# Row maxima negated on ScalarE and 1e-9 added on GpSimd, instead of on VectorE, in a top-32 attention with PReLU MLP and switch MoE

## What is computed

```python
scores = scale * np.matmul(q, k.transpose(0, 1, 3, 2))      # (4, 8, 576, 576), scale = 1/8
kth = np.partition(scores, -32, axis=-1)[..., -32:-31]
scores = np.where(scores >= kth, scores, -1000000000.0)
scores = scores - np.max(scores, axis=-1, keepdims=True)
attn = np.exp(scores)
attn = attn / (np.sum(attn, axis=-1, keepdims=True) + 1e-09)
x = heads_side_by_side(np.matmul(attn, v))                  # (2304, 512)
h = x @ w_in                                                # (2304, 2048)
x = (np.maximum(h, 0.0) + alpha * np.minimum(h, 0.0)) @ w_out
# then a switch MoE: rows with x @ w_skip > 0 go through one of 8 experts
```

## Time and profile before

| what | us |
|---|---|
| median of 3 runs (lowest, highest) | 1212.34 (1211.54, 1213.21) |
| the profiled execution's own time | 1211.7 |
| its span in the trace | 1209.8 |
| VectorE busy | 954.1 (79% of the span) |
| TensorE busy with matmuls | 944.9 (78%) |
| ScalarE busy | 599.5 (50%) |
| GpSimd busy | 414.3 (34%) |

### The profile page before, as it was taken

The page is one execution under the profiler, slowest core; times in us unless marked ns, Lnnn a source line. Parts: engine busy times, 40 slices in busy tenths (PEclk is TensorE's granted clock), DMA queues, the critical chain, the costliest instruction groups (busy, mean ns, idle before and its releaser), DMA issues.

```text
span 1209.8 us, 21193 instructions
## 1 busy us (share of the span) xinstructions
PE 944.9 (78%) x6064; PEld 625.1 (52%) x6065; DVE 954.1 (79%) x2108; ACT 599.5 (50%) x1267; POOL 414.3 (34%) x541
## 2 busy tenths in 40 slices
PE   5355545448898889889888988998889998399885
PEld 3233323225575657566665756666566776144342
DVE  6899999999999999999999999999974800411111
ACT  4547444346845853684486378448536911011000
POOL 0102344645812851383176138317610000101010
PEclk9866656559999998899999999999998999599989
DMA  6435021401002001100200020020014451544630
GB/s 172 168 104 169 13 87 45 124 1 31 2 11 70 18 10 48 41 0 10 69 20 10 12 77 0 10 70 1 1 40 141 143 170 45 165 151 151 209 119 17
DMA packets 73638, 83.08 MB, mean 69 GB/s; under 512 B 47164, under 2 KB 51260, under 8 KB 72000
## 3 DMA queue, kind: packets, MB, share of 16 engines
q1 hardware_dynamic: 65920, 56.90, 15.8%
q10 hardware_dynamic: 4464, 13.40, 3.2%
q0 software_dynamic: 3152, 11.54, 2.8%
HBM read 71.59 MB, written 11.53 MB: 69 GB/s over the span
## 4 chain that ended last, share of the span: by engine, by line
issue 30%; PE 28%; DVE 28%; ACT 5%; DMA 4%; DVEq 3%; POOL 1%; ACTq 0%; SPq 0%; POOLq 0%
DVE arena L1010 8%; DVE best L989 8%; DVE arena L1002 7%; PE acc L558 7%; PE acc L545 5%; PE sc L662 3%; DMA arena<-in_moe_w_dram 3%; PE sc L497 3%; PE pt_full L729 2%; DVEq L20 2%; ACT arena L865 1%; PE pt_full L515 1%; PE acc L526 1%; ACT arena L793 1%; PE pt_full L737 1%
## 5 line engine op out<-in xcount | busy, mean ns | idle before, releaser
L989 DVE MAX8 best<-arena 128x8 f32<-128x576 f32 x576 | 403.5, 742 | 6.3 <-issue 3.4
L1002 DVE MATCH_REPLACE8 arena<-best,arena 128x576 f32<-128x576 f32 x432 | 315.8, 738 | 0.0
L1274 POOL TENSOR_SCALAR arena<-arena,row_inv 128x576 f32<-128x576 f32 x144 | 105.1, 745 | 384.5 <-DVE row_inv L1022 384.5
L545 PE MATMUL acc<-arena 128*128 (+1 forms) x1536 | 203.5, 289 | 24.9 <-ACT neg_part L832 19.4
L515 PE MATMUL pt_full<-ident,arena 128*128 128x128 f32 x576 | 109.8, 323 | 130.1 <-POOL arena L1274 76.5
L558 PE MATMUL acc<-arena 128*128 128x288 f16 x1472 | 201.0, 289 | 0.0
L545 PEld LDWEIGHTS acc<-arena 128*128 128x128 f16 x1536 | 147.8, 99 | 76.5 <-issue 33.0
L558 PEld LDWEIGHTS acc<-arena 128*128 128x128 f16 x1472 | 144.0, 99 | 43.6 <-issue 8.0
L515 PEld LDWEIGHTS pt_full<-ident,arena 128*128 128x128 f32 x576 | 76.3, 163 | 170.5 <-issue 86.0
L1010 DVE SCALAR_TENSOR_TENSOR arena<-arena,best 128x576 f32<-128x576 f32 x144 | 150.1, 1089 | 5.7 <-ACT arena L793 5.7
L786 ACT ACTIVATE arena<-sc 128x576 f32<-128x576 f32 x144 | 92.3, 644 | 106.8 <-PE sc L497 89.2
(11 more groups left out here) (160 smaller groups left out, 1019.9 us busy)
## 6 DMA issues: line engine op xcount, KB each, us to landing
arena<-in_moe_w_dram SPq DMA_DIRECT2D x64, 512.0 KB, 3.6
arena<-in_v_dram ACTq DMA_DIRECT2D x4, 1152.0 KB, 6.2
x_rows<-x2n SPq DMA_DIRECT2D x24, 192.0 KB, 2.5
out_dram<-x2n SPq DMA_DIRECT2D x24, 192.0 KB, 2.6
nat<-in_q_dram SPq DMA_DIRECT2D x32, 128.0 KB, 2.5
nat<-in_v_dram SPq DMA_DIRECT2D x32, 128.0 KB, 2.1
arena<-in_moe_w_in_dram ACTq DMA_DIRECT2D x4, 1024.0 KB, 5.1
arena<-in_moe_w_out_dram ACTq DMA_DIRECT2D x4, 1024.0 KB, 5.8
```

The source lines that it names most:

```text
L545: last = nc.tensor.matmul(dst[:, 0:HALF], win16[:, a, d, f * P:(f + 1) * P], xT16[:, bass.ds(row + d, 1), b, bass.ds(col, HALF)].rearrange ...
L989: nc.vector.max(best[:, gp, j, r, :], src).then_inc(max_found if r == 0 else dve_step, 1)
L1002: nc.vector.match_replace(left[:, j, :], best[:, gp, j, r, :], src, MASKED).then_inc(dve_step, 1)
L1274: nc.gpsimd.tensor_scalar(probs[:, gp, j, :], probs[:, gp, j, :], row_inv[:, gp, j:j + 1], 1.0, ALU.mult, ALU.mult)\
```

## The change

Three things are changed, in four functions. In `exps` ScalarE itself makes `neg_max`, with an ACTIVATE of type Copy and the scale -1/8; it waits for the group's three first MAX8 (`max_found`) and not for VectorE's step. In `normalise` GpSimd itself makes `row_den`, with a TENSOR_SCALAR of 128 x 3; it waits for the group's last SCALAR_TENSOR_TENSOR (`dve_step`). VectorE loses both steps; its RECIPROCAL stands behind all three first MAX8 of the next search instead of behind the second, and waits for GpSimd (`den_ready`). GpSimd still waits for the RECIPROCAL before it multiplies.

```diff
--- before.py
+++ after.py
@@ -332,6 +332,7 @@
             f = (n - DT) * (FT1 // OUT_CHUNKS)
             return wout16[:, a, f:f + FT1 // OUT_CHUNKS, :].rearrange("p f n -> p (f n)")
 
+        SEARCH_STEPS = GROUP * (2 * ROUNDS - 2) + GROUP
         PARTS = 2 * GROUP * (GROUPS - 1)
         assert PARTS % DT == 0
         LEAK_STEPS = 2
@@ -788,6 +789,8 @@
 
             def exps(p, par, g):
                 gp = (GROUPS * par + g) % 2
+                act.wait_ge(max_found, GROUP * (GROUPS * p + g + 1))
+                nc.scalar.activation(neg_max[:, gp, :], best[:, gp, :, 0, 0], ACT.Copy, scale=-SCALE).then_inc(neg_max_ready, 1)
                 act.wait_ge(neg_max_ready, GROUPS * p + g + 1)
                 for j in range(GROUP):
                     nc.scalar.activation(probs[:, gp, j, :], scores[:, GROUP * g + j, :], ACT.Exp,
@@ -989,8 +992,8 @@
                         nc.vector.max(best[:, gp, j, r, :], src).then_inc(max_found if r == 0 else dve_step, 1)
                         if r:
                             steps.used += 1
-                        elif j < 2 and not first:
-                            invert(GROUPS * p + g - 1, 1 - gp, steps.base + steps.used, j)
+                    if r == 0 and not first:
+                        invert(GROUPS * p + g - 1, 1 - gp)
                     if r == ROUNDS - 1:
                         break
                     for j in range(GROUP):
@@ -1001,9 +1004,6 @@
                             hold(dve, dve_step, steps.base + steps.used - GROUP + 1)
                         nc.vector.match_replace(left[:, j, :], best[:, gp, j, r, :], src, MASKED).then_inc(dve_step, 1)
                         steps.used += 1
-                    if r == 0:
-
-                        nc.vector.tensor_scalar(neg_max[:, gp, :], best[:, gp, :, 0, 0], -SCALE, None, ALU.mult).then_inc(neg_max_ready, 1)
                 for j in range(GROUP):
                     hold(dve, dve_step, steps.base + steps.used - GROUP + 1)
                     hold(dve, exp_ready, TILES * p + GROUP * g + j + 1)
@@ -1012,16 +1012,11 @@
                                                    accum_out=row_sum[:, gp, j:j + 1]).then_inc(dve_step, 1)
                     steps.used += 1
 
-            def invert(n, gp, masked, part):
-
-                if part == 0:
-                    hold(dve, dve_step, masked)
-                    nc.vector.tensor_scalar_add(row_den[:, gp, :], row_sum[:, gp, :], 1e-9).then_inc(den_ready, 1)
-                else:
-                    hold(dve, den_ready, n + 1)
-                    nc.vector.reciprocal(row_inv[:, gp, :], row_den[:, gp, :]).then_inc(inv_ready, 1)
-
-            SEARCH_STEPS = GROUP * (2 * ROUNDS - 2) + GROUP
+            def invert(n, gp):
+
+                hold(dve, den_ready, n + 1)
+                nc.vector.reciprocal(row_inv[:, gp, :], row_den[:, gp, :]).then_inc(inv_ready, 1)
+
             linked = [0]
 
             def link_scale(ins):
@@ -1098,8 +1093,7 @@
                         search(2 * i + par, par, g, steps)
                 assert steps.used == 2 * GROUPS * SEARCH_STEPS
             done = [STEPS * 2 * GROUPS * SEARCH_STEPS]
-            for part in range(2):
-                invert(GROUPS * PAIRS - 1, (GROUPS * PAIRS - 1) % 2, done[0], part)
+            invert(GROUPS * PAIRS - 1, (GROUPS * PAIRS - 1) % 2)
 
 
             for m in range(HALVES - MLP_LAG, HALVES):
@@ -1269,6 +1263,8 @@
 
             def normalise(p, par, g):
                 n, gp = GROUPS * p + g, (GROUPS * par + g) % 2
+                hold(pool, dve_step, SEARCH_STEPS * (n + 1))
+                nc.gpsimd.tensor_scalar(row_den[:, gp, :], row_sum[:, gp, :], 1e-9, 1.0, ALU.add, ALU.mult).then_inc(den_ready, 1)
                 hold(pool, inv_ready, n + 1)
                 for j in range(GROUP):
                     nc.gpsimd.tensor_scalar(probs[:, gp, j, :], probs[:, gp, j, :], row_inv[:, gp, j:j + 1], 1.0, ALU.mult, ALU.mult)\
```

## The result

| | before | after |
|---|---|---|
| median of 4 runs (lowest, highest), us | 1211.94 (1207.74, 1213.21) | 1247.98 (1247.36, 1251.13) |
| ratio, with its 95% interval | | 1.0309 (1.0278 to 1.0340) |
| profiled execution, span, us | 1211.7, 1209.8 | 1247.36, 1245.5 |

The change makes the kernel 3.1% slower. The forecast was 1237, or +24.8; measured are +36.0 between the medians and +35.7 between the spans. The direction was right, and so was the place of the loss at the stops, but 11 us more were lost than forecast, and most of these elsewhere.

The account below looks back on a forecast made before the run. The prediction took VectorE to bound the kernel until 900 us. Its terms, 33.2 - 12.8 + 3.9 + 0.5 = +24.8 us on the profiled 1211.7, gave 1236.5, stated as 1237 because the runs' median stood 0.6 higher; range 1222 to 1248.

Parts of the forecast that it names:

- the stops: Two places per turn, twelve in all, where VectorE was to wait at the RECIPROCAL for GpSimd, late with leak.
- Term 3: The first twelve slots and slot 12: a longer ring in slots 6 to 11, less small wins; +3.9 us.
- Term 1: The twelve stops of the six turns: VectorE waits at the RECIPROCAL for GpSimd's late row_den; +33.2 us.
- Term 2: From each turn's second stop to the next turn's head: VectorE's slots return to undisturbed length; -12.8 us.
- Term 4: Behind the last search: the trip over GpSimd has no cover; +0.5 us.
- small prices: Assumed costs in the chain, such as GpSimd's step 0.2 us (0.1 to 0.5) and ScalarE's instruction 0.3 (0 to 0.4).
- the first rival: GpSimd's chain from a turn's first to third normalisation shrinks as TensorE and ScalarE catch up; 1226 or 1222 us; 15%.
- the third turn's 1.5: 1.5 us taken off Term 1, since the third turn's exponentials are late and ScalarE will have caught up.
- the ring: Slots 6 to 11: normalisation, transposes, exponentials, GpSimd's weight subtraction, VectorE's last step; longer by 0.65 + 0.3 us in five slots.
- a sign of being wrong: VectorE waiting for ScalarE at L1010, RECIPROCAL waits outside the twelve stops (and 207 us), or a chain under 40 us.
- Only the ports count: Rival: two port-blocked instructions leave VectorE and the wait for GpSimd costs nothing; about 1192 us; 4%.
- ScalarE's step: ScalarE's 48 added instructions, about 14 us in all, are hidden, apart from 0.3 us a turn in GpSimd's chain.

Follow-up runs that it names:

- b1: The changed kernel with the RECIPROCAL behind the second round of MAX8 at the two late stops of each turn; 1231.7 us, 1.0171.
- a2: The changed kernel with neg_max put back on VectorE, so only row_den and the RECIPROCAL differ from before; 1247.1 us, 1.0299.
- c1: The changed kernel with 12 spare matmuls on TensorE in the routing block of each turn; 1239.4 us, 1.0232 against before.
- c2: The kernel before with 12 spare matmuls on TensorE in the routing block of each turn; 1207.0 us, 0.9961.
- b4: The changed kernel with each turn's 16 blocks of leak cut 3, 6, 7 behind its first three normalisations, instead of 5, 7, 4; 1264.6 us, 1.0449.
- a1: The kernel before with only neg_max moved to ScalarE; 1211.6 us, 1.0007.
- a4: The kernel before without row_den: the RECIPROCAL takes row_sum itself, behind the second MAX8 as before; 1206.8 us, 0.9958.
- b3: The kernel before with neg_max on ScalarE and row_den made nowhere, the RECIPROCAL taking row_sum; 1208.4 us, 0.9887.
- a3: The kernel before with only the RECIPROCAL moved behind the third MAX8, row_den still on VectorE; 1216.2 us, 1.0048.
- c3: The kernel before with row_den made nowhere and 12 spare matmuls in each turn's routing block; 1195.7 us, 0.9872.
- d1b: The kernel before with neg_max on ScalarE, row_den made nowhere and 12 spare matmuls in each turn's routing block; 1190.8 us, 0.9828.

## Where the prediction held, and where it failed

I compare shifts of the searches' moments, after less before. A turn's head is the moment of its second search, where the first of the two slots with stops begins (13, 19 and so on).

| | predicted | measured |
|---|---|---|
| Term 3, up to search 13 (282.64 - 278.22) | +3.9 | +4.4 |
| Term 1, the six pairs of slots with the stops | +33.2 | +31.6 |
| Term 2, between the stops | -12.8 | -3.1 |
| Term 4, end | +0.5 | +0.1 |
| work behind the last normalisation (unchanged code) | 0 | +2.7 |
| sum | +24.8 | +35.7 |

The median, 1248, lies at the upper end of the forecast's range, which was set there for term 2 halved and small prices high. The small prices came out as assumed and Term 2 at a quarter, with 2.7 us more from elsewhere, so that this end was met is luck.

**Term 1 held.** The first turn's pair costs 325.85 - 314.81 - 4.42 = 6.62, the others 4.48, 3.72, 4.88, 6.21 and 5.67. The waits are 4.00 to 5.52 us at the first stop (said: 3 to 5) and 1.77 or 1.78 at the second (said: 0.5 to 2), 39.0 in the twelve; the prediction's "near 30" for their sum was too low by its own terms, since VectorE wins something in the same slots. The chain behind the turn's first normalisation is 326.02 - 282.89 = 43.1 us long, 41.6 before, so it didn't shrink; in the six turns it is 43.1, 41.2, 41.7, 41.2, 41.7 and 41.7, never under the 40 that the prediction named, and the first rival is out. (That rival's own sum is 10 us beyond the third turn's 1.5 and not 11.) The trip itself costs what was assumed: 0.20 for the step and 0.45 us until GpSimd goes on. That the queue, and not the trip, is the cause was only argued in the prediction; b1's trace shows it, and a2 that nothing else of the change is needed for the loss.

**Term 3 held**, and by the ring it named. One more detail: GpSimd's `row_den` stands behind the subtraction of the weights, at two of the first twelve groups. The second:

```profile
209.30 4.06 POOL L1289 TENSOR_TENSOR arena<-arena 128x2048 f16<-128x2048 f32 x1
213.65 0.80 POOL L372 DMA_DIRECT2D arena<-in_moe_w_out_dram  x1 [0.30 <-POOL arena L1289]
214.53 0.19 POOL L1267 TENSOR_SCALAR row_den<-row_sum 128x3 f32<-128x3 f32 x1
```

```profile
214.76 0.18 DVE L1018 RECIPROCAL row_inv<-row_den 128x3 f32<-128x3 f32 x1 [5.43 <-POOL row_den L1267]
```

Where the long `row_den` of the earlier trace rows was blocked by the subtraction for 3 us, VectorE now waits 5.4 for the subtraction, the DMA's issue and the step. The port's price was replaced by a queue's. The other of the two places, 5.23 us at 153.09, is one that the prediction didn't name and that it had listed as a sign of being wrong; Term 3's total holds it.

**Term 2 failed**, by 9.7 us, and that is the step on which the forecast broke: it gave VectorE all of the 12.8 us back, because ScalarE's exponentials were said to be mostly ready some us before they are wanted. The 12.8 were what VectorE's four slots had over undisturbed ones (the figures listed add up to 12.7), and the blocks of `leak` would be over earlier. They are: the three SCALAR_TENSOR_TENSOR of the first of these slots take 2.28 us instead of 3.27, as forecast. But the cover was gone at three places, and 8.2 us went into the three new waits for exponentials. The prediction had named this, a wait for ScalarE at L1010, as a sign of being wrong. The turns show it one by one. The forecast was about 68 us for these four slots of the first turn. After needs 68.2 and 68.3 in the second and fourth turn, and 71.0, 70.7 and 71.6 in the first, third and fifth, which end in the waits.

With the routing block filled (c1) the same stretches are 6.5 us shorter than in after, and of the 8.2 us of waits 1.7 are left. As the spare matmuls win 1.9 there in the kernel before, too (c2), Term 2 between c1 and c2 is -7.8. So of the 9.7, 6.5 hang on the block that the spare matmuls fill, and TensorE's half clock behind it is what changes there; for the other 3.2, of which 1.7 are waits for exponentials, no run shows the cause.

What made the clock fall for longer in these turns stays open. It isn't ScalarE's extra instruction alone: a2, without it, has long stretches behind the second and fourth turn's block, and before has one. Nor is it the idle time in front of the block, 0.68 us in all the 50 turns, the first of before among them, where the clock stayed at 1.00. By the Trainium skill ("TensorE: Matmul & The Clock Gate", HAM oscillation) a matmul loop that waits long enough between groups begins each group throttled; the trace agrees at 343.7 (3.34 us of waiting, then 0.50), though curing that place was worth nothing, and the costly one, behind the narrow matmuls, has only 0.68 us of idle time in front.

**The tail** of +2.7 us isn't the change's: between the last normalisation and the end the kernels here take from 307.8 (c2) to 317.8 us (b4), before 310.2, after 313.0, in code that is the same for all. It should have stood in the range as scatter.

**"Only the ports count"** is out: the two steps' ports were freed, and the time rose. The Trainium skill ("Perfetto Trace Analysis", Optimizing Scalar/DVE Operations) says that moving work between GpSimd and VectorE might not help, for their shared port's sake. The result agrees and the reason is another here: the queue's order, 50.1 us of waits in 15 places.

**ScalarE's step** was costed at nothing beyond 0.3 in the chain. That holds in the time (a1, 1.0007; a2 against after), though not in the waits: without it the loop has 4.7 us of waits for exponentials and not 8.5. a1 also shows that the 7.4 us which `neg_max` cost VectorE can't be had while exponentials are the next limit.

## What to carry to other kernels

Before a small step goes to another engine to relieve the one that bounds the kernel, read what stands directly ahead of it in that engine's order wherever that engine is late; its lateness costs nothing until the busy engine must wait for it, and then costs all of itself. If it must go there, collect the result later (b1), or drop the step (a4). When VectorE is the bound and its successor is near, count a microsecond taken off it as won only as far as the next engine's results are early, and look at TensorE's clock in those slots: how long it stays down behind the same block can differ from turn to turn.

## What the runs showed that I had not expected

Twelve spare matmuls in the routing block, 72 in all over six turns, made three kernels faster: after from 1.0309 to 1.0232, before to 0.9961, a4 from 0.9958 to 0.9872. For the fourth, b3 from 0.9887 to 0.9828, the intervals overlap. 24 matmuls of 9 columns in 2.18 us, with short idle times around them, were followed in the first turn of after by nearly 7 us at 1.2 GHz, with TensorE busy all the time, and in the first turn of before by none. Which of the two the spare matmuls cure, the narrow matmuls or the idle times around them, wasn't separated, since they fill both.

Putting work off can slow down the engine that makes it: with `leak` two or three blocks later, ScalarE waited 27.0 us for empty buffers, and the kernel lost another 17 us.

The RECIPROCAL of 128 x 3 was never held up by GpSimd's work, in none of 48 places in after (at most 178 ns) as in before (176), while the TENSOR_SCALAR of the same size took up to 3336 ns before. In these two traces no large GpSimd instruction ran all through a RECIPROCAL. In a4 one did, at the very search of the long `row_den`:

```profile
205.27 4.44 POOL L1288 TENSOR_TENSOR arena<-arena 128x2048 f16<-128x2048 f32 x1
```

```profile
207.06 0.15 DVE L1018 RECIPROCAL row_inv<-row_sum 128x3 f32<-128x3 f32 x1
```

So it is the operation: where `row_den` stood for 3.34 us, the RECIPROCAL took 0.15. In six of the traces (a1, a3, a4, b3, c3, d1b) 39 RECIPROCALs ran wholly inside a longer GpSimd instruction, and none of them took over 172 ns.
